# Running the first MoE 512 tokens at a time, in two steps a slice, inside a fused attention and MoE kernel

## The reference, cut to what matters

```python
def _attn_ref(r, k, v, w, u):            # (4, 8, 768, 48) each: batch, heads, tokens, width
    for t in range(S):
        cur = einsum('bhd,bhe->bhde', u * k[t], v[t])
        y[t] = einsum('bhd,bhde->bhe', r[t], state + cur)
        state = w[t][..., None] * state + einsum('bhd,bhe->bhde', k[t], v[t])

def _moe_ref(x, w1, w2, w3, w_out):      # x (3072, 384), w1, w2 (384, 1024), w3 (1024, 1024), w_out (1024, 384)
    return ((x @ w1) * (x @ w2)) @ w3 @ w_out

def _moe2_ref(x, w_gate, w1, w2):        # 8 experts, w1 (8, 384, 1024), w2 (8, 1024, 384)
    P = exp(x @ w_gate - max);  8 rounds of P /= row sums, P /= column sums, P *= N / 8
    return sum(P[:, e:e+1] * (maximum(x @ w1[e], 0) @ w2[e]) for e in range(8))
```

## Time and profile before

| | us |
|---|---|
| median of 3 runs | 2097.84 |
| lowest and highest run | 2094.7 and 2102.64 |
| time of the profiled execution | 2096.77 |
| its span, first to last instruction | 2094.9 |
| TensorE busy in it | 2016.7 |
| VectorE, ScalarE, GpSimd busy | 1206.2, 860.1, 603.3 |
| first attention and MoE stage, up to the first matmul of the second MoE | 542.0 |

### The profile page before, as it was taken

How to read it: one execution, slowest core, us unless ns; L and a number is a source line. 1 busy time by engine, 2 the same in 40 slices (tenths; PEclk the granted TensorE clock), 3 DMA queues, 4 the chain that set the end, 5 groups by cost and what they waited for, 6 DMA issues and landing times.

```text
span 2094.9 us, 39841 instructions
## 1 busy us (share of the span) xinstructions
PE 2016.7 (96%) x16047; PEld 1684.5 (80%) x16047; DVE 1206.2 (58%) x1879; ACT 860.1 (41%) x1577; POOL 603.3 (29%) x661
## 2 busy tenths in 40 slices
PE   7999999999898999999979999999999999999998
PEld 4699999999777777877768888888877877788887
DVE  3666666654586676666664545554464554455554
ACT  4555555554444444444433333333342333333332
POOL 2111111113555776666640111111041110111111
PEclk9999999999999999999989999999999999999999
DMA  8411211200343755666533444344443334344532
GB/s 206 84 44 36 57 44 34 57 14 15 136 171 118 246 176 177 209 204 187 164 132 131 146 167 160 137 150 142 151 140 129 128 142 170 135 157 132 163 128 101
DMA packets 116294, 273.61 MB, mean 131 GB/s; under 512 B 10192, under 2 KB 73616, under 8 KB 108048
## 3 DMA queue, kind: packets, MB, share of 16 engines
q1 hardware_dynamic: 115424, 270.59, 40.3%
q10 hardware_dynamic: 688, 0.48, 0.1%
HBM read 198.58 MB, written 71.27 MB: 129 GB/s over the span
## 4 chain that ended last, share of the span: by engine, by line
PE 60%; issue 24%; POOL 7%; DVE 4%; DMA 2%; ACT 1%; SPq 0%; POOLq 0%; DVEq 0%; ACTq 0%
PE ps L1485 13%; PE ps L1487 12%; PE ps L1486 12%; PE ps L1289 6%; PE ps L1290 5%; PE ps L1291 5%; POOL x L630 3%; PE ps L1362 3%; PE ps L1312 2%; POOL late_sum L627 1%; PE ps L1401 1%; PE ps L1403 1%; DVE xs_lo L1041 1%; DVE h_lo L1222 1%; POOL x L716 1%
## 5 line engine op out<-in xcount | busy, mean ns | idle before, releaser
L1487 PE MATMUL ps<-h_hi,w 128*128 128x512 f32 x1152 | 456.6, 396 | 0.0
L1485 PE MATMUL ps<-h_hi,w 128*128 128x512 f32 x1152 | 455.3, 395 | 0.0
L1486 PE MATMUL ps<-h_lo,w 128*128 128x512 f32 x1152 | 452.1, 392 | 0.0
L977 ACT ACTIVATE h_hi<-tb 128x512 fp32r<-128x512 f32 x378 | 238.7, 633 | 467.1 <-DVE tb L1218 239.0
L763 ACT ACTIVATE tb<-ps 128x512 f32<-128x512 f32 x378 | 226.8, 600 | 458.3 <-PE ps L1487 453.2
L630 POOL TENSOR_TENSOR x<-x,tmp 128x512 f32<-128x512 f32 x126 | 171.3, 1379 | 734.4 <-DVE tmp L1235 733.4
L1214 DVE TENSOR_TENSOR tb<-tb,ps 128x512 f32<-128x512 f32 x252 | 172.0, 685 | 270.8 <-PE ps L1487 261.1
L1222 DVE SCALAR_TENSOR_TENSOR h_lo<-tb,h_hi 128x512 fp32r<-128x512 f32 x378 | 297.3, 788 | 52.0 <-ACT h_hi L977 45.8
L1218 DVE TENSOR_TENSOR tb<-ps,tb 128x512 f32<-128x512 f32 x252 | 173.4, 689 | 219.8 <-PE ps L1487 218.9
L1486 PEld LDWEIGHTS ps<-h_lo,w 128*128 128x128 f32 x1152 | 220.7, 192 | 50.3
L1487 PEld LDWEIGHTS ps<-h_hi,w 128*128 128x128 f32 x1152 | 217.6, 189 | 47.2
(11 more groups left out here) (159 smaller groups left out, 3119.1 us busy)
## 6 DMA issues: line engine op xcount, KB each, us to landing
w<-w_rows SPq DMA_DIRECT2D x128, 384.0 KB, 5.0
early<-early_rows SPq DMA_DIRECT2D x42, 1024.0 KB, 4.8
late<-late_rows SPq DMA_DIRECT2D x42, 896.0 KB, 4.6
w_rows<-w SPq DMA_DIRECT2D x64, 384.0 KB, 6.1
early_rows<-early SPq DMA_DIRECT2D x21, 1024.0 KB, 6.2
late_rows<-late SPq DMA_DIRECT2D x21, 896.0 KB, 4.7
w_raw<-w SPq DMA_DIRECT2D x32, 576.0 KB, 5.8
Pb<-p_rows SPq DMA_DIRECT2D x24, 512.0 KB, 9.7
```

The source lines that it names most:

```text
L977: nc.scalar.activation(h_hi[:, b, :], tb[:, t_of(G, b), :], ACT.Relu).then_inc(h_hi_made, 1)
L1485: mm(o, w_hi, x_hi, start=start, stop=False, skip_group_check=True)
L1486: mm(o, w_hi, x_lo, start=False, stop=False, skip_group_check=True)
L1487: return mm(o, w_lo, x_hi, start=False, stop=stop, skip_group_check=True)
```

## The change

Two units make a twin: a slice is now a twin (512 tokens) and one block f, so there are 48 slices, and each takes two steps. In its first step (half = 0) `go_up(n, 0)` makes a, 9 matmuls of 512 columns, and in its second (half = 1) `go_up(n, 1)` makes b, in the same one PSUM bank (`UP_BANK`), which is free for b once `copy_a` has read a, and for the next slice once `make_ab` has read b. `ab`, `ab_hi` and `ab_lo` have one buffer of 512 columns. `go_down(n, d)` is one output block, 3 matmuls of 512: blocks 0 and 1 of slice n - 1 go behind `go_up(n, 0)`, block 2 stands ahead of `go_up(n, 1)`. The slices begin at step 24 (`UP_AT`), so there are 24 + 96 = 120 steps in place of 111, and the last 24 have no attention. `make_W` takes 3 products a step, the six pieces of w1 and w2 are split at steps 16 to 21, and SP's loads of w1, w2 and w3 move with them. `x` is copied from PSUM in one go by ACT, rounded, and DVE takes the low part from PSUM as well (`split_last_y`, `take_x` at k = 5), so that POOL's rounding, `xT` and two of ACT's copies go, and `move_gap` moves high and low rows. `make_ruk` moves from k = 4, 5 to k = 6, 7. The xs tiles are made one a step over 15 steps. Several buffers move (`w1_raw`, `w2_raw`, `Pb`, `p_turned`, `Ktok` over `ruk`), and the load of `w1_raw` for the second MoE waits for the 45th of 48 slices to be down, in place of `up_done`. In group 0 ACT's order becomes: `take_ab` of the last slice, high part of h for block 0, high part of h for block 1, the last `copy_x2`, `copy_gate`, `take_late`, `take_w2`.

```diff
-    LAG = 16
+    UP_AT = 24
+    TWIN = 2 * CT
+    TWINS = U // 2
     W_FROM = 3
-    SLICES = NF * U
+    SLICES = NF * TWINS
+    STEPS = UP_AT + 2 * SLICES
...
-    W_EACH = 5
-    WAB_AT = 9
+    W_EACH = 3
+    WAB_AT = 16
+
+    LAST_X = UP_AT + 2 * NF * (TWINS - 1) + 1
...
-        up_bank = lambda n: 4 + n % 2
+        UP_BANK = 4
-        x2_ps = lambda d: ps[:, 6 + d // 2, CT * (d % 2):CT * (d % 2) + CT]
+        x2_ps = lambda d: ps[:, 5 + d, :]
...
-            sp.wait_ge(x_split, U)
-            sp.wait_ge(up_done, NF * (U - 1))
-            load_w1(0)
             sp.wait_ge(wg_set, 1)
             sp.dma_start(wg[:, :, 0:E], w_gate.rearrange("(k p) e -> p k e", p=P)).then_inc(wg_loaded, 16)
-            sp.wait_ge(down_done, NF * (U - 1) + 3)
+            sp.wait_ge(down_done, down_no(SLICES - NF + 3))
             load_first(0)
-            sp.wait_ge(down_done, SLICES)
+            sp.wait_ge(down_done, down_no(SLICES - NF + 5))
+            load_w1(0)
+            sp.wait_ge(down_done, down_no(SLICES))
...
-                act.wait_ge(up_done, n + 1)
-                if n >= 2:
-                    act.wait_ge(ab_split, n - 1)
-                copy(ab[:, n % 2, :], ps[:, up_bank(n), 0:CT]).then_inc(a_copied, 1)
+                act.wait_ge(up_done, 2 * n + 1)
+                if n:
+                    act.wait_ge(ab_split, n)
+                copy(ab[:, :], ps[:, UP_BANK, :]).then_inc(a_copied, 1)
 
             def take_ab(n):
                 act.wait_ge(ab_made, n + 1)
-                if n >= 2:
-                    act.wait_ge(down_done, n - 1)
-                copy(ab_hi[:, n % 2, :], ab[:, n % 2, :]).then_inc(ab_hi_made, 1)
+                if n:
+                    act.wait_ge(down_done, down_no(n))
+                copy(ab_hi[:, :], ab[:, :]).then_inc(ab_hi_made, 1)
...
-            for s in range(SLICES + LAG - 1):
+            for s in range(STEPS):
                 u, k = divmod(s, NF)
-                n = s + 1 - LAG
+                n, half = divmod(s - UP_AT, 2)
+                if n >= 1 and half == 0:
+                    take_ab(n - 1)
                 if u < U and k >= 1:
                     pad(u, k - 1)
-                if n >= 0:
+                if n >= 0 and half == 0:
                     copy_a(n)
...
+                if n >= NF:
+                    q, f = divmod(n - NF, NF)
+                    if (f, half) == (0, 1):
+                        copy_x2(q, 0)
+                        copy_x2(q, 1)
+                    if (f, half) == (1, 0):
+                        copy_x2(q, 2)
+                if s - 1 in GATE_AT:
+                    copy_gate(GATE_AT[s - 1])
+                if s == LAST_X:
+                    act.wait_ge(up_done, LAST_X - UP_AT)
+                if 0 <= s - LAST_X < NP:
+                    take_xs(0, X_FIRST[s - LAST_X])
...
+                        take_ab(SLICES - 1)
                     take_first_h(G, 0)
-                    if st == 0:
-                        copy_x2(U - 1)
                     take_first_h(G, 1)
                     if st == 0:
+                        for d in range(KD):
+                            copy_x2(TWINS - 1, d)
                         copy_gate(NT - 1)
+                        take_late(1)
...
+            def split_last_y(u):
+                dve.wait_ge(y_copied, u + 1)
+                dve.wait_ge(x_copied, u + 1)
+                low_part(yT[:, 1, :], y_ps[:, CT * LAST:CT * PAIRS], yT[:, 0, :]).then_inc(y_split, 1)
+
             def take_x(u):
-                dve.wait_ge(x_hi_made, u + 1)
-                low_part(x_lo[u % 2][:, :, :], xT[:, :, :], x_hi[u % 2][:, :, :]).then_inc(x_split, 1)
+                x = x01[u // 2 % 2]
+                low_part(x[:, 1, :, x_cols(u)], y_ps[:, 0:CT * LAST].rearrange("p (g t) -> p g t", t=CT), x[:, 0, :, x_cols(u)]).then_inc(x_split, 1)
...
+                dve.wait_ge(up_done, 2 * n + 2)
                 dve.wait_ge(a_copied, n + 1)
-                ve.tensor_tensor(ab[:, n % 2, :], ps[:, up_bank(n), CT:2 * CT], ab[:, n % 2, :], ALU.mult).then_inc(ab_made, 1)
+                ve.tensor_tensor(ab[:, :], ps[:, UP_BANK, :], ab[:, :], ALU.mult).then_inc(ab_made, 1)
 
             def split_ab(n):
                 dve.wait_ge(ab_hi_made, n + 1)
-                low_part(ab_lo[:, n % 2, :], ab[:, n % 2, :], ab_hi[:, n % 2, :]).then_inc(ab_split, 1)
+                low_part(ab_lo[:, :], ab[:, :], ab_hi[:, :]).then_inc(ab_split, 1)
...
+                ab_due = n >= 1 and half == 0
+                if ab_due:
+                    make_ab(n - 1)
                 if u < U:
                     if k == 0:
                         set_near(u)
                     else:
-                        level(u, k - 1)
-                if 1 <= u <= U and k == 6:
-                    take_x(u - 1)
-                if n >= 0:
-                    make_ab(n)
+                        level_r(u, k - 1)
+                if ab_due:
+                    split_ab(n - 1)
+                if u < U and k:
+                    level_k(u, k - 1)
+                if 1 <= u <= U:
+                    if k == 5:
+                        split_last_y(u - 1)
+                        take_x(u - 1)
                 for f in W_in(s):
                     split_W(f)
                 if 0 <= s - WAB_AT < 2 * KD:
...
                 if 1 <= u <= U:
                     if k in (1, 2) and keyed(u - 1, k - 1):
                         next_state(u - 1, k - 1)
-                if u + 1 < U and k in (4, 5):
-                    make_ruk(u + 1, k - 4)
-                if n >= 0:
-                    split_ab(n)
-                if s >= SLICES + 7:
-                    i = 2 * (s - SLICES - 7)
-                    for p in X_FIRST[i:i + 2]:
-                        split_xs(0, p)
+                if u + 1 < U and k in (6, 7):
+                    make_ruk(u + 1, k - 6)
+                if 0 <= s - LAST_X < NP:
+                    split_xs(0, X_FIRST[s - LAST_X])
...
+            def go_up(n, m):
+                q, f = divmod(n, NF)
+                if m == 0:
+                    if n == 0:
+                        pe.wait_ge(wab_split, 2 * KD)
+                        pe.wait_ge(w3T_copied, 2 * NF)
+                    else:
+                        pe.wait_ge(ab_made, n)
+                    if f == 0:
+                        pe.wait_ge(gap_moved, GAP_MOVE * (2 * q + 2))
+                else:
+                    pe.wait_ge(a_copied, n + 1)
                 cols = slice(P * f, P * f + P)
-                for m in range(2):
-                    o = ps[:, up_bank(n), CT * m:CT * m + CT]
-                    for k in range(KD):
-                        last = split_product(o, wab_hi[:, m, k, cols], wab_lo[:, m, k, cols],
-                                             x_hi[u % 2][:, k, :], x_lo[u % 2][:, k, :], k == 0, k == KD - 1)
+                x = x01[q % 2]
+                for k in range(KD):
+                    last = split_product(ps[:, UP_BANK, :], wab_hi[:, m, k, cols], wab_lo[:, m, k, cols],
+                                         x[:, 0, k, :], x[:, 1, k, :], k == 0, k == KD - 1)
                 last.then_inc(up_done, 1)
 
-            def go_down(n):
-                u, f = divmod(n, NF)
+            def go_down(n, d):
+                q, f = divmod(n, NF)
                 if n == 0:
                     pe.wait_ge(W_split, NF)
-                pe.wait_ge(ab_split, n + 1)
-                if f == 0 and u:
-                    pe.wait_ge(x2_copied, KD * u)
-                for d in range(KD):
-                    cols = slice(P * d, P * d + P)
-                    last = split_product(x2_ps(d), W_hi[:, f, cols], W_lo[:, f, cols], ab_hi[:, n % 2, :], ab_lo[:, n % 2, :],
-                                         f == 0 and d != 1, f == NF - 1, shared=True)
-                last.then_inc(down_done, 1)
+                if d == 0:
+                    pe.wait_ge(ab_split, n + 1)
+                if f == 0 and q:
+                    pe.wait_ge(x2_copied, KD * (q - 1) + d + 1)
+                cols = slice(P * d, P * d + P)
+                split_product(x2_ps(d), W_hi[:, f, cols], W_lo[:, f, cols], ab_hi[:, :], ab_lo[:, :],
+                              f == 0, f == NF - 1).then_inc(down_done, 1)
...
-                if 0 <= n + 1 < SLICES:
-                    go_up(n + 1)
+                if n >= 1 and half:
+                    go_down(n - 1, 2)
+                if n >= 0:
+                    go_up(n, half)
                 if 1 <= u <= U:
                     if k == 0:
                         turn_keys(u - 1)
...
                         update(u - 1)
                     if k == 3:
                         make_y(u - 1)
-                if n >= 0:
-                    go_down(n)
-                if n in GATE_AT:
-                    gate(GATE_AT[n])
-                if n - 1 in GATE_AT:
-                    turn_gate(GATE_AT[n - 1])
+                if n >= 1 and half == 0:
```

(33 more changed lines are left out.)

149 lines of the change are left out of this document (63 added, 86 removed).

## The result

The changed kernel takes 2124.65 us in the median of four runs (2121.99 to 2131.57), the kernel before 2098.22 beside it (2094.7 to 2102.64). The ratio is 1.013, with an interval of 1.0098 to 1.0162: slower by 1.0 to 1.6%. Forecast were 2106, range 2092 to 2120. The profiled execution was the slowest of the four, 2131.57 us with a span of 2129.8.

What follows compares the result with a forecast made beforehand. TensorE was taken to bound the kernel beside and behind attention, each matmul's pitch and new wait counting in full. -9 + 10 + 1.5 + 0.4 + 2.7 + 3 = +8.6 us gave a median of 2106, range 2092 to 2120.

Steps and rivals of the forecast that it cites:

- Step 4: Preparation ahead of the first slices: TensorE's idle time, 4.7 us before, was to grow by 2.7 us.
- The ring: Preparation steps that split w1 and w2: ACT and DVE's chain before the next level, 4.9 us, 7.7 us idle.
- Step 5: Passage into the second MoE: later copies and loads were to add 3 us, with nothing changed behind that.
- first term: Group 0 of the second MoE: `copy_x2` behind block 1's high part delays the last gate, +2.3 us.
- Step 3: Under the attention: single bank's waits +3.8 us, less 1.8 for matmul changes and 1.65 idle, +0.4 us in all.
- sign of being wrong: TensorE's idle time under the attention exceeding 5 us was to show the prediction wrong.
- changes between kinds of matmuls: Under the attention: 18 fewer changes between kinds of matmuls at 0.1 us, -1.8 us.
- Steps 1 and 2: First MoE: wider matmuls at 0.230 us, -9 us; one bank in the last 24 steps, +10 us, DVE +1.5.
- rivals c and d: First MoE's wide matmuls: c, 0.213 to 0.216 us, 2086 us, chance 0.08; d, no gain per column, 2115, 0.05.
- The 1.5 us for DVE's instructions on xs: Last 24 steps: DVE's instructions, slower while POOL sums, no longer fit everywhere, +1.5 us (0 to 4).
- Rival a: Preparation: the ring doesn't bind, 7.7 us less, 2099 us; chance 0.15.
- Rival b: Under the attention: the single bank's wait stays open, +12 to +15 us, 2119 us; chance 0.16.

Runs made afterwards that it cites:

- f1: Changed kernel with the preparation's loads of w1 and w2 cut to 64 of 1024 columns, the rest zeros: 2114.14 us, 1.0084 of the kernel before.
- g3: The changed kernel run again unaltered, for a second profile: 2126.51 us, 1.0147 of the kernel before.
- f4: Changed kernel with DVE making the low parts of w1 and w2 one step later: 2123.28 us, 1.0121 of the kernel before.
- f3: Changed kernel with late's high part and the last x2 taken ahead of block 1's high part in group 0: 2124.03 us, 1.0128 of the kernel before.
- g2: Changed kernel with each 512-column matmul of the first MoE made as two of 256 in the same bank: 2136.55 us, 1.0193 of the kernel before.

## Why the prediction was wrong

**Step 4 failed, the preparation at +2.7 us.** It said "TensorE's work is the same, only its idle time counts", and "the loads that SP moves each arrive steps before their use". The loads did arrive in time (no wait of TensorE there ends on a DMA). What came late was TensorE's own program, behind them. Forecast were 4.7 + 2.7 = 7.4 us of idle in the preparation, measured are 16.1, and 4.8 without the traffic (f1). The two stops and what hangs on them cost 14.0 us in the first profile, by f1, and 10.5 by the medians. I had seen the kernel before stop 1.8 us on "issue" there without asking what it was, and counted a queue only for the data in it. The ring, the part of step 4 that was worked out most closely, was right: step 24 was forecast 36.9 us after step 16 and came after 38.2, the idle time of these steps 7.7 and in g3 7.1 (at full clock), of which f4 gave back 4.6.

**Step 5 was too small, +3 for +8.** Its first term stood (2.3 us forecast ahead of the gate, 2.15 measured; the smaller ones were not measured by themselves), but "Behind that nothing changes" did not hold. `take_late` pushed POOL's low part of late back, and POOL's all-reduce came 7.6 us behind it. And behind the stop of 5.79 us the matmuls start 0.43 us apart (589.00 and 589.42 in the trace), at half clock. f3 gave back 7.1 of the 8.

**Step 3 was too small, +0.4.** The attention ends at 467.6 us; of the 7.5 us of idle up to 480, 1.9 are the first two waits of the slices that follow. Under the attention TensorE is idle for 5.6 us, just over the 5 that the prediction named as a sign of being wrong. I had 3.8, all at the bank (18 places at 0.2 are in fact 3.6). The waits of TensorE from 124.7 to 467 us:

```profile
PE ps L1309 <- DVE ab_lo L1042: 2.2, 8, 0.3
PE ps L1309 <- DVE ab L1133: 1.4, 3, 0.6
```

The second is the bank. Besides these three places it shows in seventeen of 0.09 or 0.14 us, too short for this view, 1.9 us together. So the bank costs 3.3 us, near the forecast in sum, but in a shape that was not forecast. The first is `go_down` waiting for the split of ab, 0.4 to 0.5 us more than the usual 0.23 from start to start in each of eight places, and I had called that wait covered. The 1.8 us that step 3 takes off for changes between kinds of matmuls were not measured.

**Steps 1 and 2 held in the main.** The pitch is 0.231 us in the median (g2 gives 7.2 us for the width, forecast were 9), so rivals c and d are out. (Rival c says that the stage moves a third of the second MoE's data; by the earlier trace rows it is 42 against 177 GB/s, a quarter.) The bank costs 1.18 us from start to start in five of the last slices, as laid out, and 0.91 behind a `turn_gate`; `update` did not cover it in one place where that was forecast. TensorE is idle for 8.5 us from 467.6 us to the second MoE. The 1.5 us for DVE's instructions on xs show in one place, with 0.1 us. Rival a is out, since the ring binds. Rival b, a bank wait open under attention at 12 to 15 us, gave a time near the measured one, but by a mechanism that isn't there: the bank costs 3.3 us under the attention.

The sum over the profile: forecast end of the first MoE 542 - 9 + 11.5 + 0.4 + 2.7 = 547.6; measured 564.4, 16.8 more. f1 takes 13.8 of it. The other 3 lie behind the first up; step 3's 5.6 us of idle in place of 3.8 are part of them, the rest is not divided. The passage adds 5, which makes 21.8 over the forecast; the median lies 2124.65 - 2106 = 18.7 over it. The other 4.4 us of this profile lie behind 640 us and are absent from g3's.

## What to carry to other kernels

A long unrolled program is itself traffic on the DMA engines. Where a stop stands in the middle of a run of equal instructions and ends on nothing, count the instructions ahead of it and compare with another run: if the stops stand at the same counts, look at what is queued ahead of the instruction packets, and hand large loads out in pieces at the pace at which they are used. When work moves on one engine, follow it to the next engine's next instruction, most of all to a POOL routine that needs microseconds of its own ahead of it. Edits that each seem worth nothing in the median can still add up when they lie one behind the other.

## What the runs showed of the hardware

TensorE's program came in packets of 16,384 bytes, one for 125 matmuls. Behind queued loads TensorE stopped for up to 6.2 us (g2) at the border of a block, 475, 600, 727, 853, 979 or 1106 matmuls from the start, and went on 1.3 to 1.7 us after the packet had landed. The same program stopped at two of these borders for over 4 us in one execution and only at the second in another. After the stop that ended at 49.2 us TensorE ran at 1.2 GHz (granted 0.50 from 50 to 53 us): three products of `make_W` took 2.29 us, where six take 2.20. A high share of busy DMA engines alone doesn't do it: the kernel before had them busy at 0.9 or more from 36 to 66 us, but for one slice of 0.9 us, and stopped for 1.8 us. What decides when a block is asked for was not settled. POOL's all-reduce started 6.2 to 8.3 us behind POOL's last instruction ahead of it, in thirteen traces.
